# Attention with two MLPs: the last token block, the rms scales and their bank drains moved to other units

## The chip, the cores and the metric

The kernel runs on one core of a Trainium2 chip. The metric is the device time of one execution in microseconds (us), lower is better. The engines are TensorE (PE in the profile, PEld its weight loads), VectorE (DVE), ScalarE (ACT), GpSimd (POOL) and SyncE (SP, here only a DMA queue).

## The reference

Pairs of queries are averaged, attention runs on them, and the result, 1152 tokens of 512, goes through two MLPs.

```python
q_pool = q.reshape(B, H, S // 2, 2, D).mean(axis=3)          # B 2, H 8, S 1152, D 64
attn = softmax(q_pool @ k.T / 8);  x = attn @ v              # -> x: 1152 x 512
# MLP1, d_ff 2048
h = x @ w_in
g = (a0 + a1 h + a2 h^2 + a3 h^3) / (1 + |b0||h| + |b1|h^2 + 1e-6)
x = g @ w_out
# MLP2, d_ff 1536
rms = sqrt(mean(x * x, axis=-1) + 1e-6)
xn = x / rms * rms_g
out = (silu(xn @ w_gate) * (xn @ w_val)) @ w_out
```

All is float32. Products are taken in split form: each operand is a high part and a low part (what is left of it), and three matmuls (high-high, low-high, high-low) stand for one.

## The kernel before

The program is written engine by engine. Each engine has its own list of instructions, run in order, and semaphores are the only link between them: `wait_ge(s, n)` holds an engine until n has been counted on s, `.then_inc(s, k)` counts when an instruction ends. No scheduler reorders anything, so the place of a call in an engine's list is its place in time.

Attention fills the first 280 us, MLP1 the time to 482 us, MLP2 the rest. Both MLPs work on units: a unit is one of 4 blocks of 128 hidden channels (f) of a chunk of 512, for one of 3 column blocks (nb) of 384 tokens. MLP2 has 3 chunks of 12 units, counted by m from 0 to 35. Its 1152 tokens are 9 token blocks of 128 (t from 0 to 8), so three token blocks make a column block. MLP2's units 0 to 3 use column block 0, units 4 to 7 block 1, units 8 to 11 block 2.

A unit of MLP2 is this chain. PE runs `first_product` (line 645 on, matmuls at L641): 12 matmuls for the gate, 12 for the value, into two PSUM banks. VectorE multiplies the gate by the rms scales of the tokens (L1127, tile `rrow`), ScalarE takes Silu (L914), VectorE scales the value (L1129) and multiplies (L1132), ScalarE writes the high part (`gt_hi`, L922), VectorE the low part (`gt_lo`, L1134). Unit m's banks are used again by unit m+2, which waits for L1132 of m. Behind some units PE runs a `second_product` (L682), the product with w_out of one token block. The first of MLP2 stands behind unit 6.

Two things have to be made between MLP1 and MLP2, and they are spread over the first units of MLP2:

- The tokens, transposed. PE transposes a token block (`turn_tokens`, L635, four transposes), VectorE multiplies by rms_g (`tokens_scale`, L1093), ScalarE copies the high part (`tokens_hi`, L817), VectorE takes the low part (`tokens_lo`, L1021). Unit 4 needs token blocks 3 to 5, unit 8 needs 6 to 8.
- The scales 1/rms, as a row. ScalarE sums squares, VectorE takes the mean (`mean_square`, L1074), ScalarE does Ln and Exp (`root`, L877 and L879), VectorE one Newton step in four operations (`newton_root`, L1081 to L1087), PE turns the three columns (`turn_scales`, L621), ScalarE copies the row out of PSUM (`row_copy`, L883). Set n (0, 1, 2) serves column block n, so set 2 is wanted by VectorE in unit 8.

All these turns of PE share two PSUM banks, `xb0` and `xb1`, in turn. `TURNS` gives their order; "x" n+9 is token block n for MLP2 and "r" n is set n of the scales. Its end is: tokens 3, 4, 5, 6, scales 1, tokens 7, tokens 8, scales 2. `bank_free` makes a turn wait until the turn two places ahead of it in this order has been drained: by `tokens_lo` for tokens (semaphore xt_lo), by `row_copy` for scales (row_done). So tokens 8 wait for row_copy(1), scales 1 and tokens 7 for the low parts of tokens 5 and 6, scales 2 for the low part of tokens 7.

GpSimd splits the weights of later chunks into high and low parts (`split_w`, L429 and L431), a piece at a time as they come by DMA.

Of the kernel before, what the change touches and what calls it, by code (L numbers as in the profile page):

```python
# [79 lines left out]
def build(nc, q, k, v, w_in, w_out, a, b, w_gate, w_val, w_out2, rms_g, out):  # L80
# [3 lines left out]
    with top:  # L84
# [399 lines left out]
        def _(pe):  # L484
# [130 lines left out]
            def turn_scales(n):  # L615

                pe.wait_ge(rms_v, 6 * n + 6)
                bank_free(("r", n))
                for j in range(BT):
                    t = BT * n + j  # L620
                    ins = nc.tensor.transpose(rbank(n)[:, P * j:P * j + P], rfin[:, t:t + 1].to_broadcast([P, P]), ident[:])  # L621
                ins.then_inc(row_t, 1)

            def turn_tokens(t, mlp2):

                n = t + (TILES if mlp2 else 0)
                if mlp2:
                    pe.wait_ge(acc_done, TILES * (NC1 - 1) + t + 1)
                else:
                    pe.wait_ge(rows_done, PAIRS + (t >= 4))  # L630
                    if t == 0:
                        pe.wait_ge(pt_lo, 27 * PAIRS - 3)
                bank_free(("x", n))
                for d in range(DK):
                    ins = nc.tensor.transpose(xbank(n)[:, P * d:P * d + P], tok[:, t, P * d:P * d + P], ident[:])  # L635
                ins.then_inc(xt_t, 1)
# [83 lines left out]
            for u in range(UNITS * NC1, UNITS * (NC1 + NC2)):  # L720
                first_product(u)
                m = u - UNITS * NC1
                if m == 0:
                    turn_scales(0)
                    second_product(*left[2])
                if m == 1:
                    second_product(*left[3])
                    turn_tokens(3, True)
                    second_product(*left[4])
                    turn_tokens(4, True)  # L730
                if m == 2:
                    turn_tokens(5, True)
                    turn_tokens(6, True)
                if m == 3:
                    turn_scales(1)
                    turn_tokens(7, True)
                if m == 4:
                    turn_tokens(8, True)
                if m == 7:
                    turn_scales(2)  # L740
                for c, t in behind(u, NC1):
                    second_product(c, t)
# [5 lines left out]
        def _(act):  # L748
# [62 lines left out]
            def tokens_hi(t, mlp2):  # L811
                n = t + (TILES if mlp2 else 0)
                if mlp2:
                    act.wait_ge(xt_scaled, t + 1)
                else:
                    act.wait_ge(xt_t, n + 1)
                nc.scalar.activation(xt[0][:, :, P * t:P * t + P], xbank(n)[:].rearrange("p (d n) -> p d n", d=DK), ACT.Copy).then_inc(xt_hi, 1)  # L817
# [5 lines left out]
            for c in range(1, NCH):  # L823
                act.wait_ge(prep_t, c + 1)
                m = [m for kind, m in CHUNKS[c] if kind == "k"]
# [48 lines left out]
            def root(n):  # L874
                col = slice(3 * n, 3 * n + 3)
                act.wait_ge(rms_v, 6 * n + 1)
                nc.scalar.activation(lnm[:, col], mean[:, col], ACT.Ln, scale=2.0 ** -M_SHIFT).then_inc(rms_s, 1)  # L877
                act.wait_ge(rms_s, 2 * n + 1)
                nc.scalar.activation(rinv[:, col], lnm[:, col], ACT.Exp, bias=rms_bias[:], scale=-0.5).then_inc(rms_s, 1)  # L879

            def row_copy(n):
                act.wait_ge(row_t, n + 1)
                nc.scalar.activation(rrow[:, BLOCK * n:BLOCK * n + BLOCK], rbank(n)[:, 0:BLOCK], ACT.Copy).then_inc(row_done, 1)  # L883
# [24 lines left out]
            for m in range(UNITS * NC2):  # L908
                u = UNITS * NC1 + m
                c, nb, f = u // UNITS, u % UNITS // CHUNK, u % CHUNK  # L910
                act.wait_ge(gate_done, m + 1)
                if m >= 2:
                    act.wait_ge(g_lo, u - 1)
                nc.scalar.activation(silu[m % 2], hb[2 * (m % 2)][:, 0:BLOCK], ACT.Silu).then_inc(silu_done, 1)  # L914
                if m == 3:
                    row_copy(1)
                if m == 7:
                    row_copy(2)
                act.wait_ge(g_full, u + 1)
                if f == 0:  # L920
                    act.wait_ge(s2_done, TILES * (c - 1) + BT * (nb + 1))
                nc.scalar.activation(gt[0][:, f, BLOCK * nb:BLOCK * nb + BLOCK], silu[m % 2], ACT.Copy).then_inc(g_hi, 1)  # L922
                if m == 0:
                    square(6)
                if m == 1:
                    tokens_hi(3, True)
                    square(7)
                    tokens_hi(4, True)
                    square(8)
                if m == 2:  # L930
                    tokens_hi(5, True)
                    tokens_hi(6, True)
                if m == 3:
                    tokens_hi(7, True)
                if m == 4:
                    tokens_hi(8, True)
                    root(2)


        @block.vector  # L940
        def _(dve):
# [75 lines left out]
            def tokens_lo(t, mlp2):  # L1017
                n = t + (TILES if mlp2 else 0)
                dve.wait_ge(xt_hi, n + 1)
                col = slice(P * t, P * t + P)  # L1020
                nc.vector.tensor_tensor(xt[1][:, :, col], xbank(n)[:].rearrange("p (d n) -> p d n", d=DK),  # L1021
                                        xt[0][:, :, col].bitcast(F32), ALU.subtract).then_inc(xt_lo, 1)
# [48 lines left out]
            def mean_square(n):  # L1071
                col = slice(3 * n, 3 * n + 3)
                dve.wait_ge(ssq_done, 3 * n + 3)
                nc.vector.tensor_scalar(mean[:, col], ssq[:, col], 1.0 / D, RMS_EPS, ALU.mult, ALU.add).then_inc(rms_v, 1)  # L1074
# [14 lines left out]
            def tokens_scale(t):  # L1089

                dve.wait_ge(xt_t, TILES + t + 1)
                bank = xbank(TILES + t)[:].rearrange("p (d n) -> p d n", d=DK)
                nc.vector.tensor_tensor(bank, bank, g_col[:].unsqueeze(2).to_broadcast([P, DK, P]), ALU.mult).then_inc(xt_scaled, 1)  # L1093
# [25 lines left out]
            for m in range(UNITS * NC2):  # L1119
                u = UNITS * NC1 + m  # L1120
                c, nb, f = u // UNITS, u % UNITS // CHUNK, u % CHUNK
                col = slice(BLOCK * nb, BLOCK * nb + BLOCK)
                s = silu[m % 2]
                gate, val = (hb[2 * (m % 2) + j][:, 0:BLOCK] for j in range(2))
                dve.wait_ge(s1_gate, m + 1)
                dve.wait_ge(row_done, nb + 1)
                nc.vector.tensor_tensor(gate, gate, rrow[:, col], ALU.mult).then_inc(gate_done, 1)  # L1127
                dve.wait_ge(s1_done, u + 1)
                nc.vector.tensor_tensor(val, val, rrow[:, col], ALU.mult).then_inc(val_done, 1)  # L1129
                dve.wait_ge(val_done, m + 1)  # L1130
                dve.wait_ge(silu_done, m + 1)
                nc.vector.tensor_tensor(s, val, s, ALU.mult).then_inc(g_full, 1)  # L1132
                dve.wait_ge(g_hi, u + 1)
                nc.vector.tensor_tensor(gt[1][:, f, col], s, gt[0][:, f, col].bitcast(F32), ALU.subtract).then_inc(g_lo, 1)  # L1134
                if m == 0:
                    newton_root(1)
                    accumulate(NC1 - 1, 6, False)
                if m == 1:
                    accumulate(NC1 - 1, 7, False)
                    tokens_scale(3)  # L1140
                    tokens_lo(3, True)
                    accumulate(NC1 - 1, 8, False)
                    tokens_scale(4)
                    tokens_lo(4, True)
                if m == 2:
                    tokens_scale(5)
                    tokens_scale(6)
                    tokens_lo(5, True)
                    tokens_lo(6, True)
                if m == 3:  # L1150
                    tokens_scale(7)
                    tokens_lo(7, True)
                    mean_square(2)
                if m == 4:
                    tokens_scale(8)
                    tokens_lo(8, True)
                if m == 5:
                    newton_root(2)
                for c, t in behind(u, NC1):
                    accumulate(c, t, c == NC1)  # L1160
# [21 lines left out]
```

## Time and profile before

| | us |
|---|---|
| median of 3 runs (lowest, highest) | 723.96 (723.68, 724.18) |
| the profiled execution | 724.18 |
| its span in the profile | 722.4 |
| PE busy | 708.4 (98%) |
| VectorE busy | 539.2 (75%) |
| ScalarE busy | 447.0 (62%) |
| GpSimd busy | 360.4 (50%) |

The span is from the first to the last instruction of the profiled execution; its own time is 1.78 us longer. The chain that ended last is work of PE for 91% of the span. The granted clock of PE is 1.00 of full speed in all slices. Names such as P(4), gt_hi(3) or root(2) below mean the product, the high part or the root of unit or set 4, 3 or 2.

### The profile page before, as it was taken

What the parts mean: (1) busy time and instruction counts of PE and PEld (TensorE: products, weight loads), DVE (VectorE), ACT (ScalarE), POOL (GpSimd) and SP (SyncE); (2) the same over time, 40 slices, a digit from 0 to 9 for tenths busy, and PEclk for the clock granted to TensorE, in tenths of its full rate; (3) what the DMA queues carried; (4) which work ended last, traced back from release to release, by engine and by line L of the source; (5) the groups of instructions that cost most, each with busy time, mean ns of one, the idle gap of its engine ahead of it and who ended that gap; (6) DMA issues with size and microseconds to landing.
All of it is one profiled execution on the core that took longest, in us unless ns stands there. A gap on an engine that the chain in (4) does not pass through costs nothing.

```text
span 722.4 us, 12714 instructions
## 1 busy us (share of the span) xinstructions
PE 708.4 (98%) x4285; PEld 664.0 (92%) x4285; DVE 539.2 (75%) x1006; ACT 447.0 (62%) x954; POOL 360.4 (50%) x350
## 2 busy tenths in 40 slices
PE   7999999999999999799999999999999999999998
PEld 5999999999999999699999999989999999999996
DVE  5889889898989897889889888997654444444442
ACT  5887888888888877978888888874521111111110
POOL 6553635444464482788878978965642603000000
PEclk9999999999999999999999999999999999999999
DMA  7122120202030011011011011112130110000002
GB/s 238 32 69 70 32 83 16 82 16 82 16 98 14 4 59 59 0 60 36 24 59 58 2 59 58 59 40 78 59 112 5 59 59 0 1 1 1 0 37 94
DMA packets 18621, 34.93 MB, mean 48 GB/s; under 512 B 2192, under 2 KB 3216, under 8 KB 18448
## 3 DMA queue, kind: packets, MB, share of 16 engines
q1 hardware_dynamic: 18432, 34.06, 14.7%
q8 instruction: 26, 0.43, 0.2%
q10 hardware_dynamic: 144, 0.29, 0.1%
q14 instruction: 19, 0.16, 0.1%
HBM read 31.99 MB, written 2.36 MB: 48 GB/s over the span
## 4 chain that ended last, share of the span: by engine, by line
PE 91%; ACT 4%; DVE 2%; issue 1%; DMA 1%; SPq 0%; ACTq 0%
PE hb L641 32%; PE ob L682 22%; PE sc L526 12%; PE pv_ps L550 10%; PE sc L535 9%; PE misc L499 2%; PE misc L502 1%; ACT den L842 1%; ACT num L844 1%; ACT lin L845 1%; DMA qrawA<-in_q 1%; PE pv_ps L571 0%; PE misc L571 0%; PE xb L635 0%; ACT hb L861 0%
## 5 line engine op out<-in xcount | busy, mean ns | idle before, releaser
L641 PE MATMUL hb<-xt_hi,wi_hi 128*128 128x384 f32 x336 | 113.9, 339 | 4.1 <-DVE gt_lo L1060 3.8
L641 PE MATMUL hb<-xt_lo,wi_hi 128*128 128x384 f32 x336 | 113.1, 337 | 0.0
L641 PE MATMUL hb<-xt_hi,wi_lo 128*128 128x384 f32 x336 | 112.7, 335 | 0.0
L682 PE MATMUL ob<-wo_hi,gt_hi 128*128 128x512 f32 x252 | 98.6, 391 | 1.5 <-DVE gt_lo L1060 1.5
L682 PE MATMUL ob<-wo_lo,gt_hi 128*128 128x512 f32 x252 | 99.1, 393 | 0.0
L682 PE MATMUL ob<-wo_hi,gt_lo 128*128 128x512 f32 x252 | 99.0, 393 | 0.0
L966 DVE TENSOR_TENSOR pt_lo<-sc,pt_hi 128x384 fp32r<-128x384 f32 x192 | 95.0, 550 | 2.8 <-ACT pt_hi L782 1.3
L782 ACT ACTIVATE pt_hi<-sc 128x384 fp32r<-128x384 f32 x192 | 80.4, 492 | 25.7 <-PE sc L535 21.9
L768 ACT ACTIVATE prob<-sc,neg_max 128x1152 f32<-128x1152 f32 x72 | 89.5, 1243 | 1.9 <-DVE neg_max L954 1.9
L948 DVE TENSOR_REDUCE neg_part<-sc 128x1 f32<-128x768 f32 x72 | 68.9, 956 | 22.5 <-PE sc L526 22.0
L535 PE MATMUL sc<-ident,prob 128*128 128x128 f32 x648 | 82.6, 272 | 1.0 <-ACT prob L768 1.0
L535 PEld LDWEIGHTS sc<-ident,prob 128*128 128x128 f32 x648 | 75.0, 140 | 3.9 <-ACT prob L768 1.4
L471 POOL TENSOR_TENSOR num<-num,h 128x384 f32<-128x384 f32 x48 | 57.1, 1190 | 40.0 <-ACT lin L845 40.0
L914 ACT ACTIVATE silu<-hb 128x384 f32<-128x384 f32 x36 | 17.7, 492 | 93.6 <-DVE hb L1127 93.6
L641 PEld LDWEIGHTS hb<-xt_hi,wi_hi 128*128 128x128 f32 x336 | 63.1, 188 | 7.5 <-DVE gt_lo L1060 2.7
L641 PEld LDWEIGHTS hb<-xt_hi,wi_lo 128*128 128x128 f32 x336 | 63.1, 188 | 2.1
L641 PEld LDWEIGHTS hb<-xt_lo,wi_hi 128*128 128x128 f32 x336 | 63.0, 188 | 0.0
L526 PE MATMUL sc<-kqA 128*128 128x384 f32 x240 | 58.8, 349 | 2.2 <-DVE pt_lo L966 2.2
L922 ACT ACTIVATE gt_hi<-silu 128x384 fp32r<-128x384 f32 x36 | 18.9, 525 | 64.8 <-DVE silu L1132 64.8
L526 PE MATMUL sc<-kqB 128*128 128x384 f32 x240 | 58.3, 347 | 0.0
L682 PEld LDWEIGHTS ob<-wo_hi,gt_hi 128*128 128x128 f32 x252 | 47.4, 188 | 10.2 <-POOL wi_lo L431 1.7
L682 PEld LDWEIGHTS ob<-wo_lo,gt_hi 128*128 128x128 f32 x252 | 47.3, 188 | 10.1
(152 smaller groups left out, 1756.2 us busy)
## 6 DMA issues: line engine op xcount, KB each, us to landing
wraw<-in_moe_w_out SPq DMA_DIRECT2D x7, 1024.0 KB, 5.0
wraw<-in_moe_w_in SPq DMA_DIRECT2D x4, 1024.0 KB, 5.0
wraw<-in_moe_w_gate SPq DMA_DIRECT2D x3, 1024.0 KB, 5.0
wraw<-in_moe_w_val SPq DMA_DIRECT2D x3, 1024.0 KB, 5.1
krawB<-in_k SPq DMA_DIRECT2D x8, 288.0 KB, 3.7
vrawA<-in_v SPq DMA_DIRECT2D x8, 288.0 KB, 2.7
vrawB<-in_v SPq DMA_DIRECT2D x8, 288.0 KB, 2.8
qrawA<-in_q SPq DMA_DIRECT2D x8, 256.0 KB, 2.7
```

What stands on the lines that cost most here:

```text
L471: nc.gpsimd.tensor_tensor(nm[:], nm[:], h2[:], ALU.mult).then_inc(num, 1)
L526: ins = nc.tensor.matmul(sc[par][:, c, 0:KBANK], lhs, rhs, start=n == 0, stop=n == len(terms) - 1)
L535: ins = nc.tensor.transpose(sc[par][:, c, P * j:P * j + P], prob[par][:, P * m:P * m + P], ident[:])
L550: ins = nc.tensor.matmul(pv_ps[:, 0:n], v2[x][:, kt].rearrange("p a d -> p (a d)"), pt[buf][e][:, kt, c0:c0 + n], start=j == 0, stop=j == ...
L641: ins = nc.tensor.matmul(bank[:, 0:BLOCK], w[i][:, d, col], x[j][:, d, BLOCK * nb:BLOCK * nb + BLOCK], start=d == 0 and n == 0, stop=d == ...
L682: ins = nc.tensor.matmul(ob[m % 2][:], gt[i][:, f, P * t:P * t + P], wo[c % 2][j][:, f, :], start=f == 0 and n == 0, stop=f == CHUNK - 1 a ...
L768: nc.scalar.activation(prob[s][:].rearrange("p (c n) -> p c n", c=3), sc[s][:, :, 0:KBANK], ACT.Exp, bias=neg_max[:, s:s + 1], accum_out=s ...
L782: ins = nc.scalar.activation(pt[buf][0][:, 3 * c:3 * c + 3, c0:c0 + P], src, ACT.Copy)
L914: nc.scalar.activation(silu[m % 2], hb[2 * (m % 2)][:, 0:BLOCK], ACT.Silu).then_inc(silu_done, 1)
L922: nc.scalar.activation(gt[0][:, f, BLOCK * nb:BLOCK * nb + BLOCK], silu[m % 2], ACT.Copy).then_inc(g_hi, 1)
L948: nc.vector.tensor_reduce(neg_part[:, s, 0:1], sc[s][:, 0:2, 0:KBANK], AX.XY, ALU.max, negate=True).then_inc(part_done, 1)
L966: ins = nc.vector.tensor_tensor(pt[buf][1][:, kt, c0:c0 + P], src, pt[buf][0][:, kt, c0:c0 + P].bitcast(F32), ALU.subtract)
```

## The change

Calls are moved between units; none is added or left out. On PE, `turn_tokens(8)` goes from unit 4 to unit 3, directly behind `turn_tokens(7)`, and `turn_scales(2)` from unit 7 to unit 5. On ScalarE, `row_copy(1)` goes from ahead of unit 3's `gt_hi` to behind it, ahead of `tokens_hi(7)`; `tokens_hi(8)` goes from unit 4 to unit 3; `row_copy(2)` from ahead of unit 7's `gt_hi` to the end of unit 5. On VectorE, `tokens_scale(8)` and `tokens_lo(8)` go from unit 4 to unit 3, and `newton_root(2)` from unit 5 to unit 4. The order of the turns in `TURNS` stays.

```diff
--- before.py
+++ after.py
@@ -734,9 +734,8 @@
                 if m == 3:
                     turn_scales(1)
                     turn_tokens(7, True)
-                if m == 4:
                     turn_tokens(8, True)
-                if m == 7:
+                if m == 5:
                     turn_scales(2)
                 for c, t in behind(u, NC1):
                     second_product(c, t)
@@ -912,10 +911,6 @@
                 if m >= 2:
                     act.wait_ge(g_lo, u - 1)
                 nc.scalar.activation(silu[m % 2], hb[2 * (m % 2)][:, 0:BLOCK], ACT.Silu).then_inc(silu_done, 1)
-                if m == 3:
-                    row_copy(1)
-                if m == 7:
-                    row_copy(2)
                 act.wait_ge(g_full, u + 1)
                 if f == 0:
                     act.wait_ge(s2_done, TILES * (c - 1) + BT * (nb + 1))
@@ -931,10 +926,13 @@
                     tokens_hi(5, True)
                     tokens_hi(6, True)
                 if m == 3:
+                    row_copy(1)
                     tokens_hi(7, True)
+                    tokens_hi(8, True)
                 if m == 4:
-                    tokens_hi(8, True)
                     root(2)
+                if m == 5:
+                    row_copy(2)
 
 
         @block.vector
@@ -1149,12 +1147,11 @@
                     tokens_lo(6, True)
                 if m == 3:
                     tokens_scale(7)
+                    tokens_scale(8)
                     tokens_lo(7, True)
+                    tokens_lo(8, True)
                     mean_square(2)
                 if m == 4:
-                    tokens_scale(8)
-                    tokens_lo(8, True)
-                if m == 5:
                     newton_root(2)
                 for c, t in behind(u, NC1):
                     accumulate(c, t, c == NC1)
```

## Rows read from the trace of the kernel before

**Rows 1.** busy time by stretch (columns: stretch, us, busy by engine with instructions, clock, DMA)

```profile
270.00:300.00 30.00, 25.95 (x176) 24.77 (x175) 23.04 (x48) 24.15 (x52) 12.26 (x11) 1.00 0.10 36
504.00:531.00 27.00, 27.00 (x161) 26.24 (x160) 18.00 (x38) 13.20 (x22) 15.99 (x17) 1.00 0.23 79
531.00:705.00 174.00, 174.00 (x920) 163.30 (x919) 77.47 (x132) 28.50 (x56) 30.17 (x31) 1.00 0.07 24
```

**Rows 2.** TensorE's instructions in time (start, length, engine, line, operation, tiles, count), 509 to 531 us

```profile
509.94 0.42 PE L641 MATMUL hb<-xt_hi,wi_hi 128*128 128x384 f32 x1
514.19 0.60 PE L635 MATMUL xb<-ident,tok 128*128 128x128 f32 x4
514.55 0.42 PE L641 MATMUL hb<-xt_hi,wi_hi 128*128 128x384 f32 x1
518.80 0.33 PE L641 MATMUL hb<-xt_hi,wi_hi 128*128 128x384 f32 x1
522.96 0.39 PE L682 MATMUL ob<-wo_hi,gt_hi 128*128 128x512 f32 x1
529.91 0.49 PE L621 MATMUL xb<-ident,rfin 128*128 128x128 f32 x3
530.16 0.42 PE L641 MATMUL hb<-xt_hi,wi_hi 128*128 128x384 f32 x1
```

**Rows 3.** ScalarE's instructions in time, unit 3 of MLP2

```profile
510.30 0.49 ACT L883 ACTIVATE rrow<-xb 128x384 f32<-128x384 f32 x1
511.10 0.53 ACT L922 ACTIVATE gt_hi<-silu 128x384 fp32r<-128x384 f32 x1 [0.31 <-DVE silu L1132]
```

**Rows 4.** TensorE behind a wait for ScalarE, at 273 us

```profile
272.95 0.21 ACT L768 ACTIVATION_READ_ACCUMULATOR prob<-sc,neg_max 128x1 f32 x1
273.21 0.96 PEld L535 LDWEIGHTS sc<-ident,prob 128*128 128x128 f32 x9 [0.44 <-ACT prob L768]
```

**Rows 5.** unit 8 from its value product to its high part (VectorE, ScalarE)

```profile
534.63 0.57 DVE L1129 TENSOR_TENSOR hb<-hb,rrow 128x384 f32<-128x384 f32 x1 [1.51 <-PE hb L641]
535.82 0.53 ACT L922 ACTIVATE gt_hi<-silu 128x384 fp32r<-128x384 f32 x1 [2.18 <-DVE silu L1132]
```

**Rows 6.** root(2) on ScalarE with its table loads

```profile
518.32 1.28 ACT L877 ACT_TABLE_LOAD   x1
519.84 1.28 ACT L879 ACT_TABLE_LOAD   x1
521.13 0.30 ACT L879 ACTIVATE rinv<-lnm,rms_bias 128x3 f32<-128x3 f32 x1
```

**Rows 7.** newton_root(2) on VectorE, first and last operation

```profile
524.96 0.15 DVE L1081 TENSOR_TENSOR newt<-rinv 128x3 f32<-128x3 f32 x1
525.62 0.16 DVE L1087 TENSOR_TENSOR rfin<-newt,rinv 128x3 f32<-128x3 f32 x1
```

**Rows 8.** newton_root(1) on VectorE and GpSimd's weight splits beside it

```profile
493.35 0.62 POOL L429 TENSOR_SCALAR wo_hi<-wraw 128x512 fp32r<-128x512 f32 x1
493.44 0.54 DVE L1083 TENSOR_TENSOR newt<-newt,mean 128x3 f32<-128x3 f32 x1
494.01 0.17 DVE L1085 TENSOR_SCALAR newt<-newt 128x3 f32<-128x3 f32 x1
494.05 1.30 POOL L431 TENSOR_TENSOR wo_lo<-wraw,wo_hi 128x512 fp32r<-128x512 f32 x1
494.29 1.08 DVE L1087 TENSOR_TENSOR rfin<-newt,rinv 128x3 f32<-128x3 f32 x1
```

**Rows 9.** GpSimd's splits of value weights, and a low part that met a split

```profile
516.50 1.71 POOL L431 TENSOR_TENSOR wv_lo<-wraw,wv_hi 128x512 fp32r<-128x512 f32 x1
522.81 1.30 POOL L431 TENSOR_TENSOR wv_lo<-wraw,wv_hi 128x512 fp32r<-128x512 f32 x1
536.21 1.29 POOL L431 TENSOR_TENSOR wo_lo<-wraw,wo_hi 128x512 fp32r<-128x512 f32 x1
536.38 1.54 DVE L1134 TENSOR_TENSOR gt_lo<-silu,gt_hi 128x384 fp32r<-128x384 f32 x1 [0.59 <-ACT gt_hi L922]
```

## The prediction, made before the changed kernel ran

> **What bounds the kernel now.** I read the busy time by stretch first. From 504 to 531 us, where every edit lies, TensorE (PE) is busy 27.00 of 27.00 us, and 174.00 of 174.00 in the stretch behind it, up to 705 us [rows 1]. So in the second MLP nothing makes PE wait; whatever is put between two PE instructions there is paid in full at the end, and there is no idle time for a gain to come from. VectorE (18.00), ScalarE (13.20) and GpSimd (15.99) have slack in the same stretch. Then I read PE's instructions in order of time [rows 2]. Call P(m) the first product of unit m of MLP2 (24 matmuls, first gate, then value). P(4) starts at 509.94, token block 8 is transposed behind it at 514.19, P(5) starts at 514.55, P(6) at 518.80, the output product behind it at 522.96, the turning of scales 2 at 529.91 and P(8) at 530.16. A P behind another or behind an output product lasts 4.16, one behind transposes 4.25 (its first matmul is 0.09 longer), and the four transposes cost 0.36.
>
> **What the change moves.** It adds and removes no instruction. Four moves matter. (a) PE: token block 8 from behind P(4) to behind P(3). (b) ScalarE: row_copy(1), the drain of the bank with scales 1, from ahead of gt_hi of unit 3 to behind it. (c) PE: turn_scales(2) from behind P(7) to behind P(5). (d) VectorE: newton_root(2), which makes what (c) turns, from unit 5 to unit 4. The rest (VectorE's scale and low part of block 8, ScalarE's high part and row_copy(2)) moves into slack.
>
> **The first wait, (a) with (b).** The turns alternate between two banks, and bank_free makes each wait for the turn two places back. For token block 8 that is scales 1, so PE waits for row_done 2, the end of row_copy(1). Before, that copy started at 510.30, while PE had P(4) to do; the wait cost nothing. Now PE asks for it right behind token block 7, at about 509.94, where P(4) had started, and on ScalarE the copy stands behind gt_hi(3), which starts at 511.10 when the product that it copies is ready [rows 3]. Back-to-back activations here follow each other about 0.1 us before the end of the first, so the copy runs from 511.10 + 0.43 = 511.53 to 512.02. From ScalarE's last write to PE's first instruction it takes 0.05 (273.16 to 273.21) [rows 4]. So block 8 starts at 512.08, P(4) at 512.08 + 0.36 + 0.08 = 512.5 (the 0.08 is an estimate of what PE loses in starting again; the only start cost in the rows is the 0.09 of a P behind transposes), against 509.94: +2.56. P(5) then follows at 512.5 + 4.25 = 516.75 against 514.55, since block 8 no longer stands there: **+2.20 us**. Queued behind the wait on PE is everything, P(4) included; VectorE and ScalarE wait for P(4) in turn but need nothing sooner. Bounds: 2.0 if the restart is free, 2.5 if the copy starts only at the full end of gt_hi and the hand-over takes 0.2.
>
> **The second wait, (c) with (d).** turn_scales(2) needs newton_root(2), which needs root(2) on ScalarE, which stays behind gt_hi(4). I follow the chain from P(4)'s end. The value product of a unit is picked up 4.47 behind the start of a P that follows transposes (530.16 to 534.63) and gt_hi starts 1.19 later and takes 0.53 [rows 2, 5]. With P(4) at 512.5: value at 516.97, gt_hi(4) from 518.16 to 518.69. root(2) starts at 518.32 in the run before and ends at 521.13 + 0.30 = 521.43; 3.11 us, most of it two table loads of 1.28 each [rows 6]. It is then at 518.71 to 521.82. newton_root(2) is four small operations: without disturbance 524.96 to 525.62 + 0.16, so 0.82 [rows 7]. Undisturbed the scales are ready at 521.87 + 0.82 = 522.69, and PE starts to turn them at 522.74. PE finished issuing P(5) at 516.75 + 4.16 = 520.91, so it stands for at least **1.83 us**. Before, nothing waited here: the turning came 4.13 us after newton_root(2).
>
> That undisturbed price is the lower bound, because of what GpSimd does then. In [rows 8] the second of the same four operations starts at 493.44 while GpSimd splits weights (493.35 to 493.97) and ends at 493.98, 0.54 instead of 0.16; the fourth starts at 494.29 under a split until 495.35 and ends at 495.37, 1.08 instead of 0.16. An operation of VectorE with all operands in SBUF, begun during one of GpSimd's, ends only just behind it. The low part of another unit shows the same: started at 536.38 under a split until 537.50, 1.54 us [rows 9]. GpSimd splits the next value weights in 515.80 to 524.11; the last piece is at 522.81 for 1.30. These pieces hang on a DMA that the change does not move. Their times shift a little: before, gt_lo(4) collided with a piece that starts at 516.50 (1.71 instead of 1.29) [rows 9]; now that piece ends 0.42 sooner, but gt_lo(4), at 518.72, collides with the next one and holds up the third by about 0.3. I get pieces to 522.05, 522.63 and 524.0. newton_root(2)'s first operation, at 521.87, ends at 522.07 behind the first; the second behind the second at 522.65; the third slips into the gap, as the third at 494.01 did; the fourth ends at 524.02. PE turns scales 2 at 524.1. The wait is then 524.1 - 520.91 = **3.19 us**. I take this value, as the four starts fall just as in [rows 8]; the other end is 3.7, if two operations are left behind the last piece.
>
> **The rest of the sum.** Restart of PE behind the second wait 0.08, as above. turn_scales(2) itself costs the same in either place (0.25 and 0.09). Unit 5's gate on VectorE now comes behind newton_root(2), at 524.15, but its result is wanted by PE only at P(7), which stands behind P(6) and an output product, so later than 524.43 + 4.25 = 528.7, while it is there by 526. row_copy(2) comes at about 527 and is wanted in unit 8, whose P(8) was at 530.16 before and moves out too. SP's queue is not touched. Sum: 2.20 + 3.19 + 0.08 = **+5.47 us**. The profiled execution took 724.18 us (span 722.4, 1.78 around it); 724.18 + 5.47 = 729.65. The median of the runs is 0.22 below the profiled one: **729.4 us**.
>
> A rule weighed against the rows: the Trainium skill, "ScalarE: Activation LUTs", section "Table sets: the hidden batching unit", says that Ln followed by Exp needs one load, since one set holds both. Here the trace does not agree: root(2) has a load ahead of its Ln and one ahead of its Exp, 1.28 us each [rows 6]. By the rule root(2) would end 1.3 us sooner, newton_root(2) would be through before the last piece of GpSimd, and the result would be near 728.0. The rows decide.
>
> **Rivals.**
> Undisturbed newton. Both waits are there, but newton_root(2) meets no split, because GpSimd's pieces lie elsewhere. For it: the two other free copies took 0.15 to 0.17 an operation [rows 7]. Against: the splits stood until 524.11 before. Then 2.20 + 1.83 + 0.08 = 4.11, that is 728.1 us. Chance 0.16.
>
> One wait only. The scales are ready by 520.9, the second wait vanishes and only the bank costs: 2.2, so 726.2 us. It needs root(2) about 2 us sooner than its place behind gt_hi(4) allows. Chance 0.04.
>
> Clock. The granted clock is 1.00 throughout, the 2.4 GHz level, also in 270 to 300 us, where PE was idle 4.05 of 30 us [rows 1]; a single stop of 3.2 us has no row. If the clock fell to 1.2 GHz behind it, P(6) would take up to twice its 4.25, so some 4.2 more, 733.6 us. Against: no stretch here shows a fall. Chance 0.07. The Trainium skill, "TensorE: Matmul & The Clock Gate", section "Part 1: The HAM clock gate", says that an idle array drops to the lower level and needs activity to return, which speaks for this rival; no row of this case shows it.
>
> The other side: no wait at all. It would need row_copy(1) finished by 509.94 and the scales by 520.9; then only PE's merged transposes remain, which save the longer first matmul of a P (0.09) once or twice: 723.8 us, no change. It decides at row_copy(1): its start must come before gt_hi(3), as in the kernel before, and the edited order forbids it. Chance 0.04; a gain over 0.2% would need 1.45 us from an engine that has none idle.
>
> **How the numbers follow.** Forecast 0.69, rivals 0.16, 0.04, 0.07 and 0.04. About 0.2% (1.45 us) is what a measurement of this kernel tells from no change. The range leaves out the single wait, the clock and the no-wait case, and holds the undisturbed newton with its lower bound (2.0 + 1.83 = 3.8, less some spread) and the forecast's upper one (2.5 + 3.7 = 6.2): 727.6 to 730.5. Slower by over 0.2%: 0.95, the no-wait case is most of the rest: same 0.03, faster 0.02.
>
> **What would show each step.** PE's transposes of the last token block idle about 2 us behind those of block 7, released by ScalarE's copy of the scales' row at about 512.0. PE's turning of scales 2 idle about 3.2 us, released by VectorE's last newton operation, with two of the four operations stretched and ending with GpSimd's pieces. PE's busy time in all unchanged, its idle 5.4 longer, and from P(6) on each row of before some 5.4 us later. Wrong if PE has no idle row in 509 to 525, if the newton operations are all at 0.16, or if matmuls behind the second wait are at twice their length.

## The result, and the profile after

| | us |
|---|---|
| changed kernel, median of 4 runs (lowest, highest) | 731.21 (729.84, 732.37) |
| kernel before beside it, median of 4 runs | 723.89 |
| ratio, 95% interval | 1.0100 (1.0079, 1.0121) |
| profiled execution of the changed kernel, its span | 730.53, 728.7 |

The change costs 1.0%, 7.3 us. The forecast was 729.4 in a range of 727.6 to 730.5: slower as forecast, but the time lies above the range. Both waits came as worked out; a third term, the fall of TensorE's clock, which the forecast had as an unlikely rival, came on top. In the last experiment one run of 4022 us and one of 1177 us (of the kernel before) are in the medians, which they hardly move, and not in the ratio.

TensorE's waits in the changed kernel (engine, line, what it waited for: us in total, times, longest). The two `xb` rows are new; the others stand for waits of attention and MLP1 that the kernel before has too. Its longest stop anywhere is 1.7 us:

```profile
PE hb L641 <- DVE gt_lo L1058: 3.8, 3, 1.7
PE xb L621 <- DVE rfin L1085: 3.1, 1, 3.1
PE xb L635 <- ACT rrow L882: 2.0, 1, 2.0
PE ob L682 <- DVE gt_lo L1058: 1.5, 1, 1.5
```

TensorE in time, changed kernel; these answer to [rows 2]:

```profile
508.87 0.63 PE L635 MATMUL xb<-ident,tok 128*128 128x128 f32 x4
511.45 0.63 PE L635 MATMUL xb<-ident,tok 128*128 128x128 f32 x4 [1.96 <-ACT rrow L882]
511.84 0.42 PE L641 MATMUL hb<-xt_hi,wi_hi 128*128 128x384 f32 x1
516.09 0.33 PE L641 MATMUL hb<-xt_hi,wi_hi 128*128 128x384 f32 x1
523.51 0.54 PE L621 MATMUL xb<-ident,rfin 128*128 128x128 f32 x3 [3.10 <-DVE rfin L1085]
523.81 0.47 PE L641 MATMUL hb<-xt_hi,wi_hi 128*128 128x384 f32 x1
524.71 0.53 PE L641 MATMUL hb<-xt_hi,wi_hi 128*128 128x384 f32 x1
527.53 0.34 PE L641 MATMUL hb<-xt_hi,wv_hi 128*128 128x384 f32 x1
529.64 0.39 PE L682 MATMUL ob<-wo_hi,gt_hi 128*128 128x512 f32 x1
```

Token block 8 waits 1.96 us for the scales' row, the turning of scales 2 waits 3.10 us for `rfin`. (The idle time in brackets counts from the modelled end of the last matmul, which lies behind the step to the next one: by the starts, P(5) comes 2.23 us later behind token block 7 than before.) Then P(6) runs from 523.81 to 529.64, 5.83 us, where a P behind transposes lasted 4.25 [rows 2]: its first matmuls come every 0.32 us instead of 0.174. From 527.53 the step is back at 0.17. That is 1.58 us.

Busy time and granted clock by stretch, changed kernel (the third number from the right is the clock; [rows 1] had 1.00 in each stretch):

```profile
515.00:520.00 5.00, 5.00 (x31) 5.00 (x30) 2.77 (x3) 2.77 (x5) 4.51 (x5) 1.00 0.00 0
520.00:525.00 5.00, 1.90 (x10) 1.58 (x9) 3.50 (x7) 2.89 (x4) 3.27 (x4) 0.90 0.10 9
525.00:530.00 5.00, 5.00 (x23) 4.96 (x23) 1.40 (x4) 1.39 (x3) 1.25 (x2) 0.75 0.57 204
530.00:535.00 5.00, 5.00 (x27) 4.53 (x26) 3.31 (x5) 0.53 (x1) 4.83 (x6) 1.00 0.00 0
```

The clock stood at its lower level (1.2 GHz) for part of 520 to 530 and was back at 2.4 GHz by 530. TensorE had stood for 3.10 us and was running again since 523.51 when it fell: in steps of 1 us the granted clock is 1.00 up to 524, 0.52, 0.50, 0.50 and 0.77 up to 528, and 1.00 behind that. The weights that come by DMA in the same stretch are not what slows the matmuls: from 511 to 514 of the same run the DMA share is 0.75 to 1.06 with the clock at 1.00 and P(4)'s matmuls 0.17 apart.

VectorE and GpSimd in the second wait, changed kernel; these answer to [rows 7, 8]:

```profile
521.16 0.36 DVE L1079 TENSOR_TENSOR newt<-rinv 128x3 f32<-128x3 f32 x1 [1.48 <-ACT rinv L878]
521.56 0.54 DVE L1081 TENSOR_TENSOR newt<-newt,mean 128x3 f32<-128x3 f32 x1
522.13 0.17 DVE L1083 TENSOR_SCALAR newt<-newt 128x3 f32<-128x3 f32 x1
522.41 1.05 DVE L1085 TENSOR_TENSOR rfin<-newt,rinv 128x3 f32<-128x3 f32 x1
```

```profile
520.25 1.26 POOL L431 TENSOR_TENSOR wv_lo<-wraw,wv_hi 128x512 fp32r<-128x512 f32 x1
521.47 0.62 POOL L429 TENSOR_SCALAR wv_hi<-wraw 128x512 fp32r<-128x512 f32 x1
522.17 1.26 POOL L431 TENSOR_TENSOR wv_lo<-wraw,wv_hi 128x512 fp32r<-128x512 f32 x1
```

The first Newton operation ends at 521.52 with the first piece (521.51), the second at 522.10 with the second (522.09), the fourth at 523.46 just behind the third (523.43); only the one in the gap takes 0.17.

The start of MLP2 differs between executions (P(0) at 481.95 before, 481.14 after), so below I compare the time from P(0) to the end of the span: 722.4 - 481.95 = 240.45 before, 728.7 - 481.14 = 247.56 after, **+7.11 us**. Of these 1.58 are P(6)'s, which leaves 5.53; the forecast's sum was 5.47.

### The profile page after: what moved, and what is told of

The parts are those of the page before. It is cut to its first block, busy times and chain, and to the rows that moved or that the text cites. A ratio compares the mean times of both kernels' runs of the same rounds, so it can differ in the third digit from the quotient of the medians.

```text
span 728.7 us, 12714 instructions
## 1 busy us (share of the span) xinstructions
PE 710.2 (97%) x4285; PEld 665.1 (91%) x4285; DVE 542.9 (74%) x1006; ACT 446.4 (61%) x954; POOL 359.7 (49%) x350
## 4 chain that ended last, share of the span: by engine, by line
PE 86%; ACT 6%; DVE 5%; issue 2%; DMA 0%; SPq 0%; DVEq 0%; ACTq 0%
PE hb L641 29%; PE ob L682 21%; PE sc L526 12%; PE pv_ps L550 10%; PE sc L535 9%; PE misc L499 2%; PE misc L502 1%; DVE tok L1066 1%; ACT den L841 1%; ACT num L843 1%; ACT lin L844 1%; DVE xb L1091 1%; ACT squares L871 0%; PE pv_ps L571 0%; DMA qrawA<-in_q 0%
```

## The experiments

All were timed beside the kernel before. "From P(0)" is the growth of the time from P(0) to the end of the span, in the profiled run. "Clock low" counts the runs of the kernel whose mean granted clock was 0.998 or less. The kernel before had that in 4 of the 61 runs beside these (one of them the run of 1177 us), and 0.999 in 6 more, so 0.999 says little.

| kernel | median us | ratio, 95% interval | waits us | from P(0) | clock low |
|---|---|---|---|---|---|
| changed | 731.21 | 1.0079 to 1.0121 | 2.0 + 3.1 | +7.11 | 5 of 5 |
| both waits filled | 729.45 | 1.0052 to 1.0085 | none idle | +5.27 | 0 of 6 |
| first filled | 730.43 | 1.0081 to 1.0112 | 0 + 2.8 | +6.84 | 3 of 4 |
| second filled | 730.50 | 1.0074 to 1.0101 | 2.0 + 0 | +6.81 | 2 of 5 |
| tokens only | 727.50 | 1.0043 to 1.0069 | 2.0 | +3.75 | 4 of 5 |
| scales only | 732.14 | 1.0088 to 1.0123 | 5.3 | +7.62 | 6 of 6 |
| splits late | 728.32 | 1.0054 to 1.0080 | 2.0 + 1.6 | +4.15 | 2 of 6 |
| no table loads | 729.35 | 1.0061 to 1.0090 | 2.0 + 1.7 | +4.01 | 3 of 4 |
| both of these | 727.41 | 1.0022 to 1.0048 | 2.0 + 0 | +2.15 | 3 of 7 |
| copy put back | 730.52 | 1.0065 to 1.0101 | 0.75 + 4.1 | +6.93 | 5 of 6 |
| scales at unit 6 | 727.31 | 1.0025 to 1.0054 | 2.0 | +2.04 | 3 of 7 |
| copy and scales back | 725.06 | 0.9998 to 1.0018 | 0.75 | +1.18 | 0 of 12 |

The medians carry something that the change has no part in: P(0) started anywhere from 481.11 to 483.01 in the profiled runs, and the kernel before took 723.04 to 725.61 us in runs whose clock was 1.000. So differences below 2 us are read from the growth from P(0), where one run stands for each kernel, and from the rows.

**Both waits filled.** My theory (A) is that the waits cost 5.1 to 5.5 us and the clock the rest; the rival (B) that the waits themselves vary. `fill(m, n)` issues n matmuls whose result nobody reads (the comment is added here):

```diff
                     turn_tokens(7, True)
+                    fill(4, 11)      # 11 matmuls 128x384 into the bank that P(4) overwrites
                     turn_tokens(8, True)
                 if m == 5:
+                    fill(6, 17)
                     turn_scales(2)
```

> The changed kernel, with matmuls that compute nothing wanted put on TensorE in both waits: 11 ahead of token block 8's transposes, 17 ahead of the turning of scales 2, each 128x384 at 0.174 us, so 1.9 and 3.0 us of the 2.0 and 3.1 us. Theory A (two waits, and a clock that falls behind them): the waits' end times stay, so the span without clock loss, 728.7 - 1.6 = 727.1, remains, the granted clock is 1.000 in every run, and the time is 728.9 with a spread under 0.5. Theory B (the clock has no part in it, the waits themselves vary from run to run): the time stays near 731 and spreads over 2 us as in the changed kernel.

TensorE in this kernel (L721 are the filling matmuls):

```profile
511.98 0.63 PE L635 MATMUL xb<-ident,tok 128*128 128x128 f32 x4
520.78 3.11 PE L721 MATMUL hb<-xt_hi,wi_hi 128*128 128x384 f32 x17
523.88 0.54 PE L621 MATMUL xb<-ident,rfin 128*128 128x128 f32 x3
524.18 0.42 PE L641 MATMUL hb<-xt_hi,wi_hi 128*128 128x384 f32 x1
528.45 0.39 PE L682 MATMUL ob<-wo_hi,gt_hi 128*128 128x512 f32 x1
```

P(6) lasts 528.45 - 524.18 = 4.27 us again. Five of the six runs had the clock at 1.000, the sixth 0.999. The growth is 5.27 where it was 7.11: with work that is thrown away the kernel got faster by 1.84 us. 1.56 of them are P(6)'s; another 0.27 is that the scales were ready 42.05 us behind P(0) instead of 42.32, which the fillers did not bring about. By the medians it is 729.45 against 731.21, with intervals of the ratios that overlap. Theory A holds for the cause, since matmuls 0.32 us apart at a granted clock of 0.50 were there with the stops idle and gone with the stops filled; B, in which the clock has no part, falls. A's numbers were too good: the median is 0.5 above the 728.9 expected and the six times lie within 1.01 us, not 0.5.

**The two halves of the change alone.** "Tokens only" has moves (a) and (b). TensorE's part of the edit (cut; the calls of the other engines that go with it move too):

```diff
                 if m == 3:
                     turn_scales(1)
                     turn_tokens(7, True)
-                if m == 4:
                     turn_tokens(8, True)
```

> The kernel before with only moves (a) and (b): token block 8 behind token block 7 on TensorE and row_copy(1) behind gt_hi(3) on ScalarE; the scales 2 stay where they were. Both theories: one wait of 2.0 us on TensorE, time 723.9 + 2.1 = 726.0. Theory A (two waits, and a clock that falls behind them): the clock stays at 1.000 if a stop of 2.0 us alone does not bring it down; if it does, up to 2 us more and a spread. With scales alone moved the one wait was 5.3 us and the time 732.1, so here the two single edits would add to more than the change has: 2.1 + 5.3 against 5.1.

The wait was 1.96 us as expected. The time was 727.5, not the 726.0 of a full clock, and the mean clock was 0.998 in 4 of 5 runs (the fifth took 726.78). A single stop of 2.0 us is enough, and here the clock falls as soon as TensorE runs again (granted clock 1.00 up to 511, 0.86 in 511 to 512, 0.50 in 512 to 515):

```profile
511.72 1.09 PE L635 MATMUL xb<-ident,tok 128*128 128x128 f32 x4 [1.96 <-ACT rrow L882]
512.46 0.67 PE L641 MATMUL hb<-xt_hi,wi_hi 128*128 128x384 f32 x1
513.57 0.52 PE L641 MATMUL hb<-xt_hi,wi_hi 128*128 128x384 f32 x1
517.93 0.33 PE L641 MATMUL hb<-xt_hi,wi_hi 128*128 128x384 f32 x1
```

P(4) takes 5.47 us (512.46 to 517.93) instead of 4.25, and the transposes 0.74 instead of 0.36.

"Scales only" has moves (c) and (d) (cut in the same way):

```diff
-                if m == 7:
+                if m == 5:
                     turn_scales(2)
```

> The kernel before with only moves (c) and (d): turn_scales(2) behind P(5), newton_root(2) in unit 4, token block 8 left behind P(4). root(2) is then where it was in the kernel before (ends at 521.4) and GpSimd's last split ends at about 524.1, while P(5) ends at 518.8: one wait of 5.3 us. The two waits of the changed kernel (2.0 + 3.1) would then not be a sum of two costs but one due time, that of scales 2. Theory A: 723.9 + 5.4 = 729.3 and the clock's loss on top, 1.5 to 4 us, so 731 to 733. Theory B: 729.3. A theory in which each wait has its own price would give 723.9 + 3.2 = 727.1.

TensorE in this kernel, and its stretches:

```profile
523.65 0.90 PE L621 MATMUL xb<-ident,rfin 128*128 128x128 f32 x3 [5.35 <-DVE rfin L1087]
520.00:525.00 5.00, 1.34 (x6) 1.35 (x7) 2.85 (x7) 3.52 (x5) 3.02 (x3) 0.64 0.08 28
525.00:530.00 5.00, 5.00 (x22) 5.00 (x22) 1.42 (x3) 1.39 (x3) 1.37 (x2) 0.68 0.52 185
```

One wait of 5.35 us and 732.1. The change with both halves is no slower than this one: the halves are not two costs to be added. The scales are ready at 523.46 in the changed kernel and 523.59 here, and the first wait only uses up 2.2 us of the second.

That the wait came within 0.05 of the number expected is in part luck. I had it end with GpSimd's last split, but that ended at 523.11, and the last Newton operation only at 523.59: gt_lo(4) had met a split and took 1.57 us, so the high part of token block 8 and root(2) behind it came later than I took them to (root(2) ended at 521.78).

**Each wait filled alone.** The same filling matmuls in one wait, the other left idle.

> The changed kernel, with 11 unwanted matmuls of 128x384 on TensorE in the first wait only. The second wait stays an idle 3.1 us. With both waits filled the time was 729.45 (5.0 us over its own before) and the clock was at full speed; the changed kernel was 7.3 over. Theory A: the waits cost 5.1 and the rest, some 2, is the clock, which falls after a stop of TensorE. If it is the longer, second stop alone that does it, the clock here is below 1.000 in most runs and the time 730.5 to 731.5. Theory B' (both stops together are needed): the clock stays at 1.000 and the time is 729.4.

> The changed kernel, with 17 unwanted matmuls on TensorE in the second wait only; the first stays an idle 2.0 us. Moves (a) and (b) alone, with one stop of 2.0 us, had the clock below 1.000 in 4 of 5 runs. Theory A: so here too, in most runs, with 729.4 to 731 us; where the clock falls behind the first stop, P(4) is late, and so gt_hi(4) and root(2), but newton_root(2)'s end is tied to GpSimd's last split, so part of that loss is taken out of the second wait. Theory B': the clock stays at 1.000 and the time is 729.4.

Either stop alone brings the clock down in some runs, the longer one in 3 of 4 (the fourth had 0.999), the shorter in 2 of 5. In the profiled run with the first wait filled P(6) takes 5.80 us (523.53 to 529.33). That both stops are needed (B') is refuted. Where the clock fell behind the first stop (the profiled run with the second wait filled), the fillers started late, at 522.56, and ended at 525.5, after the scales had been ready: part of that kernel's +6.81 is my fillers' own, so its time says nothing of the price of the clock. Two more of its runs took 730.4 and 730.5 at a mean clock of 1.000; what made them long is not known.

**What the second wait is made of.** "Splits late" holds GpSimd's splits until VectorE has passed newton_root(2):

```diff
-                        pool.wait_ge(g_lo, UNITS * NC1)
+                        pool.wait_ge(g_full, UNITS * NC1 + 6)
```

> The changed kernel, with GpSimd's splits of the value weights of chunk 1 held until unit 5's product on VectorE is done, so that newton_root(2) meets no split. The first wait stays 2.0; newton_root(2)'s four operations take 0.16 each instead of 0.36, 0.54, 0.17, 1.05, so the second wait is 1.7 to 1.8 instead of 3.1. Time without clock loss 728.9 - 1.4 = 727.5. Theory A: as neither stop is then above 2.0 us, little or no loss of clock, 727.5 to 728. If the lock on the port had no part, the wait stays 3.1.

VectorE in this kernel:

```profile
521.37 0.16 DVE L1079 TENSOR_TENSOR newt<-rinv 128x3 f32<-128x3 f32 x1 [2.57 <-ACT rinv L878]
521.57 0.16 DVE L1081 TENSOR_TENSOR newt<-newt,mean 128x3 f32<-128x3 f32 x1
521.76 0.17 DVE L1083 TENSOR_SCALAR newt<-newt 128x3 f32<-128x3 f32 x1
522.04 0.16 DVE L1085 TENSOR_TENSOR rfin<-newt,rinv 128x3 f32<-128x3 f32 x1
```

All four at 0.16, and the wait 1.64 instead of 3.10: GpSimd's part is shown, 1.46 us (forecast: 3.19 against 1.83). The median, 728.3, was above the 727.5 to 728 expected. The clock was low in 2 of 6 runs (729.18 and 730.41 us), where I had expected little or no loss; one run took 728.89 at 1.000. The profiled run, at 1.000, grew by 4.15.

"No table loads" takes them from root(2) (the calls shortened):

```diff
-  activation(lnm, mean, ACT.Ln, ...);  activation(rinv, lnm, ACT.Exp, ...)
+  for set 2: activation(lnm, mean, ACT.Copy, ...);  activation(rinv, lnm, ACT.Identity, ...)
```

> The changed kernel with root(2) computing Copy and Identity instead of Ln and Exp, so the scales of the last 384 tokens are not the root's; its two table loads, and the one ahead of silu(5), go. The chain of scales 2 is 2.56 us shorter up to newton_root(2), which starts at about 518.6 instead of 521.2. But there it meets GpSimd's splits (to 519.2, 520.2, 521.5, 522.1, 523.4 in the changed kernel), and ends with the third of them, at about 521.5: second wait 1.2 instead of 3.1, time about 1.9 under that of the changed kernel. Without the port's part it would be ready at 519.4, ahead of P(5)'s end, and the second wait gone (-3.1).

The wait fell to 1.68, not 1.2: gt_lo(4) now stood in the way too, VectorE took the first Newton operation at 519.75 instead of 518.65, and the fourth ended at 522.24 with GpSimd's fourth piece, one piece later than I had worked out. The direction holds: 2.56 us taken out of the chain give 1.4, because the rest is held by the splits.

> The changed kernel with both parts of the second wait taken out: root(2) computes Copy and Identity instead of Ln and Exp (the scales of the last 384 tokens are not the root's), and GpSimd's splits of the value weights wait until unit 5's product on VectorE is done. The splits alone took the second wait from 3.1 to 1.6, the tables alone to 1.7. If the two are the whole of it, the scales are ready 2.56 + 1.5 us sooner than in the changed kernel, ahead of P(5)'s end, and the second wait is 0: the time is that of moves (a) and (b) with turn_scales(2) hidden, 726 with the clock at full speed, to 728 where it falls behind the first stop. If a third part is left, a wait of its size remains ahead of the turning of scales 2.

With both out, no wait is left ahead of the scales (VectorE ends `rfin` at 520.60, TensorE turns it at 521.51 without stopping) and the growth is 2.15 us, the first wait and its restart. No third part.

**Two waits or one due time.** "Copy put back" has row_copy(1) ahead of gt_hi(3):

```diff
+                if m == 3:
+                    row_copy(1)
                 act.wait_ge(g_full, u + 1)
...
                 if m == 3:
-                    row_copy(1)
                     tokens_hi(7, True)
```

> The changed kernel with row_copy(1) put back ahead of gt_hi(3) on ScalarE, as in the kernel before; TensorE's order stays. The first wait shrinks from 2.0 to about 0.8 us, since the copy then starts 0.4 behind silu(3) and not behind gt_hi(3). If each wait has a price of its own, the sum falls by 1.2 us. My theory is that scales 2 have a due time of their own: newton_root(2) cannot end before GpSimd's last split, which does not move, so the second wait grows from 3.1 to about 4.2 and the sum stays at 5.1; the time is 730 to 732, as that of the changed kernel, with the clock's loss behind the longer stop.

TensorE in this kernel:

```profile
510.53 0.63 PE L635 MATMUL xb<-ident,tok 128*128 128x128 f32 x4 [0.75 <-ACT rrow L882]
523.54 0.90 PE L621 MATMUL xb<-ident,rfin 128*128 128x128 f32 x3 [4.05 <-DVE rfin L1086]
524.09 0.67 PE L641 MATMUL hb<-xt_hi,wi_hi 128*128 128x384 f32 x1
```

The first wait gave back 1.21 us and the second took 0.95 of them; root(2) ended 0.9 sooner (520.21), and newton_root(2) still only at 523.48, with GpSimd's last split (523.46). The time was 730.5, with an interval that overlaps that of the changed kernel. In the changed kernel, moving row_copy(1) back alone gains next to nothing.

> The changed kernel with turn_scales(2) and row_copy(2) in unit 6 instead of unit 5; newton_root(2) stays in unit 4. P(6), 4.2 us, then covers the wait of 3.1, so the second wait is gone and only the first, 2.0 us, is left: 723.9 + 2.1 = 726.0 with the clock at full speed, and 726.8 to 728.5 where it falls behind the first stop, as with moves (a) and (b) alone (727.5). A rival that puts the second wait's cost on newton_root(2)'s place on VectorE and not on TensorE's order would leave 729 or more.

With turn_scales(2) and row_copy(2) one unit later the second wait is gone, so its cost hung on TensorE's order and not on newton_root(2), which stayed in unit 4. The profiled run, at full clock, grew by 2.04 us from P(0), which started late in it (483.01); three of the seven runs took 725.7, those around 728.2 had a clock of 0.997 or 0.998.

> The changed kernel with row_copy(1) ahead of gt_hi(3) again and turn_scales(2) and row_copy(2) in unit 7; what is left of the change is token block 8 behind block 7 and newton_root(2) in unit 4. The first wait is 0.75 us, as with the copy alone put back, the second is none: 723.9 + 0.8 + 0.1 = 724.8, with the clock at full speed in all runs, since the stop is shorter than those that the kernel before has at 271 to 292 us (up to 1.7). If a version of this change can be no slower than the kernel before, it is near this one; I expect none that is faster, since TensorE has no idle time there.

725.06 beside 724.52, ratio 0.9998 to 1.0018, no difference that can be told. The growth from P(0) of the profiled run is 1.18 us, above the 0.8 expected: by the starts P(5) comes 1.03 later behind token block 7, and 0.22 more lies ahead of it, between the turning of scales 1 and token block 7 (0.59 against 0.37), a step that took 0.33 to 0.60 in the kernels here. What is left of the change gains nothing: no version here beats the kernel before, and with TensorE busy for 27.00 of 27.00 us [rows 1] none was to be expected.

## Why the prediction was wrong

- **What bounds the kernel**: right. Everything put between TensorE's instructions came out at the end.
- **First wait, 2.20 us**: right. The wait was 1.96 us in the profile's count and 2.23 by the starts, which is how the forecast counted, and the copy ran directly behind gt_hi(3) (510.41, the copy at 510.84). The restart that I gave 0.08 was 0.03: block 8 to P(4) took 0.39 against 0.36.
- **Second wait, 3.19 us**: right, 3.10, or 3.27 in the forecast's count. The collision with GpSimd fell piece by piece as forecast, and splits late, no tables and both together show the two parts. One reading was not exact: [rows 9] does not show the low part ending just behind the split. It ended at 537.92, 0.42 behind it, and so did gt_lo(4) in the changed kernel (519.68 against 519.26); only operations of 128x3 end within 0.03.
- **The sum, 5.47**: right as the sum of waits: 5.53 in the profiled run without P(6)'s loss, 5.27 with the waits filled.
- **The step that failed** is the term for the clock, put at nothing: the rival "Clock" and its chance of 0.07, with the reason "no stretch here shows a fall". The forecast's sum had no such term. The clock was low in all 5 runs of the changed kernel (0.993 to 0.998). In the profiled one it cost 1.58 us, shown row by row; the medians, 7.3 us over the kernel before against 5.0 to 5.4 with the waits filled, give about 2 us, but not clear of noise. With 729.4 and 1.6 the time would have been 731.0, beside 731.21 measured. The last of the forecast's own signs of being wrong, matmuls behind the second wait at twice their length, is what came. The stretch from 270 to 300 us, which I took as evidence against, has 4.05 idle us in stops of at most 1.7, and neither of the new stops is that short. There was no row for the length that the forecast itself had worked out, and 0.07 treated that lack as a no. The Trainium skill, "TensorE: Matmul & The Clock Gate", section "Part 1: The HAM clock gate", says that an idle array drops to the lower level; the rows of the changed kernel agree (0.90 and 0.75 in 520 to 530, behind a stop of 3.10 us). I had cited it and let the quiet stretch outweigh it.
- Its price, 4.2 us, was too high as well: not a whole P at twice its length, but about half of its 24 matmuls at 0.32 us.
- **The other rivals**: newton undisturbed (728.1), one wait only and no wait at all are refuted by the first trace after.
- **The table rule**: the rows decided rightly. Two loads of 1.28 stand in the changed kernel too, at 518.02 and 519.54.

Open: why the clock falls in one run of a kernel and not in another, and for how long; no length of stop at which it begins was measured. Scales only was at 0.995 in each of 6 runs, the changed kernel between 0.993 and 0.998. The kernel before shows it at times too: in the batch with both waits filled, 2 of its 11 runs had 0.998 and took 726.3, beside a median of 724.08. The changed kernel's runs of 732.1 and 732.4 us (0.995 and 0.993) have no profile, so whether the clock fell behind both stops there is not known.

## What to carry to other kernels

Where the matrix engine has no idle time, a call moved ahead in its list gains nothing and takes on the due time of what it reads; work that time out along the other engines' lists, down to operations that another engine blocks, before moving it. Two waits in a row on one engine are not two costs: shortening the first can lengthen the second, up to the ready time of what the second wants. And when such a sum gives a stop of TensorE longer than any in the trace, take the clock's loss into the forecast, here 1.6 us for a fall, and widen the range; if the stop can't be avoided, unwanted matmuls in it were worth up to 1.8 us here.

## What the runs showed that I had not expected

- A single stop of 2.0 us went with a lowered clock in 4 of 5 runs (tokens only), one of 5.3 us in 6 of 6 (scales only). With 5.3 us the clock fell while TensorE still stood (0.68 in 521 to 522, restart at 523.65); with 2.0 and 3.1 us it fell at or behind the restart.
- At the lower level an f32r matmul of 128x384 comes every 0.32 us against 0.174, 1.84 times, and four transposes cost 0.74 against 0.36.
- Three small operations on 128x3 elements took 1.11, 0.56 and 1.24 us (copy put back) where 0.16 to 0.17 is their own time, with GpSimd's splits beside them. GpSimd's next piece started at most 0.1 us behind the last, so that in these traces no more than one such operation slipped through a gap.
